# Second feed-forward: both transposes of a pair stand together on TensorE, the start of it is reordered on VectorE and ScalarE

## The chip, the cores and the metric

One core of one Trainium2 chip. The metric is device time in microseconds (us) of one execution, median of 3 runs. The profile is of one further execution, with its own time.

## The reference, cut to what matters

The output of a decayed linear attention (4 sequences, 768 positions, 8 heads of 64, so 3072 tokens of width 512) goes through two feed-forward stages. The second is the one that the change touches most:

```python
def _moe2_ref(x, w_in, w_out, g_ln):        # x 3072x512, w_in 512x1024, w_out 1024x512
    h = x @ w_in
    h_max = np.max(h, axis=-1, keepdims=True)
    e = np.exp(h - h_max)
    sm = e / (np.sum(e, axis=-1, keepdims=True) + 1e-09)
    solu = h * sm
    mu = np.mean(solu, axis=-1, keepdims=True)
    var = np.mean((solu - mu) ** 2, axis=-1, keepdims=True)
    ln = (solu - mu) / np.sqrt(var + 1e-06) * g_ln
    return (ln @ w_out).astype(np.float32)
```

The first one is `h = x @ w_in` (512 to 2048), ELU, `@ w_out`.

## The kernel before

Every engine has its program written out by hand; engines meet only at semaphores, and each engine works through its own list in order. So what stands ahead of an instruction in the list can hold it up even where its data are there. Matrix products are made in split precision: an operand is kept as a high half (ScalarE copies it) and a low half (GpSimd or VectorE subtracts), and each product is three matmuls. Up-projections use Winograd's form of Strassen's scheme: seven block products instead of eight, with sums before (GpSimd on the data, VectorE on the weights) and after.

The stages: attention in 12 steps; the first feed-forward in 3 blocks of 512 tokens by two, with 8 rounds `n` in each (`quadrants`, lines 882 and 1173; `up_pair` on TensorE); the second feed-forward in 12 pairs `u` of 128-token tiles `t` = 2u and 2u+1. Between the last two stages lies a passage, in which the last down-products of the first stage, the first pairs of the second and the writing back of results are woven by hand.

One pair `u` of the second feed-forward:

- TensorE makes seven block products of 6 matmuls each (128x512). In `opening_products` (L675): P1 (A11 B11) into PSUM bank X (4), P6 (S2 T2) into bank Y (5). In `middle_products` (L684): P2 (A12 B21) into X, P5 (S1 T1) into bank W (6), P7 (S3 T3) into Y. In `last_products` (L693): P4 (A22 T4) into Y, P3 (S4 B22) into W.
- ScalarE copies X after P1 (`copy_p1`, L1215) and after P2 (`copy_h2`, L1222). VectorE makes five sums out of SBUF and PSUM (`add`, L946): U2 from Y after P6, U3 from Y after P7, H22 = U3 + W after P5 (these three are `first_sums`, L948), H21 from Y after P4, H12 = U2 + W after P3 (`last_sums`, L958). P7 may not start before U2 has been read out of Y, P4 not before U3, P3 not before H22.
- For each tile: VectorE takes the row maximum (L978), ScalarE the exponential (L1235), VectorE the product (L985), statistics (L991 to L1005), GpSimd one power of -1/2 (`rstd`, L524), VectorE the normalisation (L1012 to L1016) into `e3`. TensorE transposes the tile in 8 transposes of 128x128 into banks 0 and 1 (`norm_transposes`, L743), ScalarE copies the high half out (`normalised_hi`, L1245), VectorE the low half (`normalised_lo`, L967), and TensorE multiplies with the second weight (`solu_down`, L757 to L759: two quarters `q` of 12 matmuls each for a tile).

TensorE's loop over p (L763) treats pair p+1's up-products together with pair p's tiles t = 2p, t+1. Its order before: opening and middle products of pair p+1; transposes of t; last products of p+1; transposes of t+1; four `solu_down` quarters. VectorE's order in the loop (L1041): `first_sums(p+1)`, low halves of t, `last_sums(p+1)`, maximum of t+2, low halves of t+1, maximum of t+3, then for t+2 and t+3 in turn product, statistics, normalisation. GpSimd (L536) splits the low halves of pair p+2 (L518, after ScalarE's copy L1228), sums those of p+3, and makes the two powers.

In round n = 0 of the first feed-forward, `keep_p1(1)` (ScalarE, L1171) and `keep_u2(1)` (VectorE) stand behind the high and low half of a quadrant (`split_g_hi`, `split_g_lo`); the second product of round 1 that adds to X waits for `keep_p1(1)`.

Of the kernel before, what the change touches and what calls it, by code (L numbers as in the profile page):

```python
# [6 lines left out]
B, H, S, D = 4, 8, 768, 64  # L7
# [43 lines left out]
def build(nc, units, w1, w_in2, w_out2, g_ln, tables, x_dram, x2_dram, out):  # L51
# [4 lines left out]
    with ctx:  # L56
# [31 lines left out]
        v_decay = place("v_decay", H, f32, CONST_AT + 32)  # L88
        state_decay = place("state_decay", H, f32, CONST_AT + 64)
# [50 lines left out]
        causal = place("causal", C, f32, E_AT + 2 * K2)  # L140
# [77 lines left out]
        v_decay_in = sem("v_decay_in")  # L218
        causal_in = sem("causal_in")
        state_decay_in = sem("state_decay_in")  # L220
# [61 lines left out]
        P1, P6, P2, P5, P7, P4, P3 = range(1, 8)  # L282
        M1, M6, M2, M7, M5, M4, M3 = range(1, 8)
        U2, U3, H22, H21, H12 = range(1, 6)
# [158 lines left out]
        def _(pool):  # L443
# [9 lines left out]
            def decay_state(s):  # L453
                pool.wait_ge(state_summed, kvs(s + 1))
                if s >= 1:

                    pool.wait_ge(att_done, s)
                nc.gpsimd.tensor_tensor(state[:, (s + 1) % 2].rearrange("p n h c -> p (n h) c"),
                                        state_sum[:, :].rearrange("p (h c) -> p h c", h=H),
                                        state_decay[:, :].unsqueeze(2).to_broadcast([P, H, D]), ALU.mult)\  # L460
                    .then_inc(state_done, 1)
# [20 lines left out]
            pool.wait_ge(state_decay_in, 16)  # L482
# [49 lines left out]
            sum_x2(2)  # L532
            split_x2_lo(2)
            rstd(0)
# [9 lines left out]
        def _(pe):  # L544
# [128 lines left out]
            X, Y, W = ps[:, 4, :], ps[:, 5, :], ps[:, 6, :]  # L673

            def opening_products(u):  # L675
                pe.wait_ge(x2l_done, 7 * (u + 1))
                if u > 0:
                    pe.wait_ge(h2_copied, u)
                up_product(u, X, A11, B11, True)
                if u > 0:  # L680
                    pe.wait_ge(h2_summed, sums(u - 1, H21))
                up_product(u, Y, S2, T2, True)

            def middle_products(u):  # L684
                pe.wait_ge(p1_copied, u + 1)
                up_product(u, X, A12, B21, False)
                if u > 0:
                    pe.wait_ge(h2_summed, sums(u - 1, H12))
                up_product(u, W, S1, T1, True)
                pe.wait_ge(h2_summed, sums(u, U2))  # L690
                up_product(u, Y, S3, T3, False)

            def last_products(u):  # L693
                pe.wait_ge(h2_summed, sums(u, U3))
                up_product(u, Y, A22, T4, False)
                pe.wait_ge(h2_summed, sums(u, H22))
                up_product(u, W, S4, B22, False)
# [39 lines left out]
            def norm_transposes(t):  # L737
                pe.wait_ge(soft[t % 2], SOFT * (t // 2 + 1))
                pe.wait_ge(nl_done, 2 * t)
                for q in range(2):  # L740
                    for f in range(NF2 // 2):
                        ff = q * (NF2 // 2) + f
                        last = nc.tensor.transpose(ps[:, q, f * P:(f + 1) * P], e3[:, t % 2, ff * P:(ff + 1) * P],  # L743
                                                   ident[:, :])
# [18 lines left out]
            for p in range(NPAIR - 1):  # L763
# [8 lines left out]
                norm_transposes(t)  # L772
                last_products(p + 1)
# [6 lines left out]
                else:  # L780
                    norm_transposes(t + 1)
# [14 lines left out]
        def _(dve):  # L796

            def apply_mask(s, one):
# [5 lines left out]
                table = causal[:, :].unsqueeze(1).to_broadcast([P, H, C])  # L804
# [40 lines left out]
            dve.wait_ge(causal_in, 16)  # L845
# [32 lines left out]
            def keep_u2(n):  # L878
                dve.wait_ge(p1_kept, n + 1)
                keep_sum(u2[:, :], n, U2, p1[:, n % 2, :], ps[:, up_bank(n // NFP) + 1, :], M6)  # L880

            def quadrants(n):
# [32 lines left out]
                split_g_lo(down_no(blk, 0, 2 * i + 1), e21)  # L915
                if n == 0:
                    keep_u2(1)
                activate(stash[:, 2 * i, :], n, G12, stash[:, 2 * i, :])
# [22 lines left out]
            X, Y, W = ps[:, 4, :], ps[:, 5, :], ps[:, 6, :]  # L941
# [6 lines left out]
            def first_sums(u):  # L948
# [3 lines left out]
                add(u3[:, :], u, U3, kept, Y, P7)  # L952
                dve.wait_ge(h2_summed, sums(u, U3))
                add(h2[:, 1, 512:1024], u, H22, u3[:, :], W, P5)
# [3 lines left out]
            def last_sums(u):  # L958

                add(h2[:, 1, 0:512], u, H21, kept, Y, P4)  # L960
                add(h2[:, 0, 512:1024], u, H12, u2[:, :], W, P3)

            def normalised_lo(t):
                for q in range(2):
                    dve.wait_ge(nh_done, 2 * t + q + 1)
                    part = slice(q * (NF2 // 2), (q + 1) * (NF2 // 2))
                    nc.vector.tensor_tensor(n_lo[:, t % 2, part, :], ps[:, q, :].rearrange("p (f t) -> p f t", t=P),  # L967
# [66 lines left out]
            add(h2[:, 1, 512:1024], 1, H22, u3[:, :], W, P5)  # L1034
            normalised_lo(0)
            solu_spread(1)
            solu_variance(1)
            add(h2[:, 1, 0:512], 1, H21, kept, Y, P4)
            solu_normalise(1)
            add(h2[:, 0, 512:1024], 1, H12, u2[:, :], W, P3)  # L1040
            for p in range(NPAIR - 1):  # L1041
                t, final = 2 * p, p == NPAIR - 2
                if p > 0:
                    if p > 1:
                        first_sums(p + 1)
                    normalised_lo(t)
                    last_sums(p + 1)
                if p > 0:
                    solu_max(t + 2)
                    normalised_lo(t + 1)  # L1050
                else:
                    normalised_lo(t + 1)
                    solu_max(t + 2)
# [8 lines left out]
                if p == 0:  # L1062

                    dve.wait_ge(p1_copied, 3)
                    add(u2[:, :], 2, U2, kept, Y, P6)
                solu_product(t + 3)
                solu_spread(t + 3)
                if p == 0:
                    add(u3[:, :], 2, U3, kept, Y, P7)
                solu_variance(t + 3)  # L1070
                if p == 0:
                    dve.wait_ge(h2_summed, sums(2, U3))
                    add(h2[:, 1, 512:1024], 2, H22, u3[:, :], W, P5)
# [6 lines left out]
        def _(act):  # L1080
            act.dma_start(v_decay[:, :], tables[:, T_VDEC:T_VDEC + H]).then_inc(v_decay_in, 16)
            act.dma_start(causal[:, :], tables[:, T_CAUSAL:T_CAUSAL + C]).then_inc(causal_in, 16)
            act.dma_start(state_decay[:, :], tables[:, T_SDEC:T_SDEC + H]).then_inc(state_decay_in, 16)
# [45 lines left out]
            act.wait_ge(v_decay_in, 16)  # L1129
# [43 lines left out]
            def quadrants(n):  # L1173
# [67 lines left out]
            def normalised_hi(t):  # L1241
                for q in range(2):
                    act.wait_ge(tr_done, 2 * t + q + 1)
                    part = slice(q * (NF2 // 2), (q + 1) * (NF2 // 2))
                    nc.scalar.activation(n_hi[:, t % 2, part, :], ps[:, q, :].rearrange("p (f t) -> p f t", t=P), ACT.Copy)\  # L1245
# [29 lines left out]
            split_x2_hi(2)  # L1275
            evacuate(NBLK - 1, 1)
            copy_p1(1)
            solu_exp(1)
            copy_h2(1)
            for p in range(NPAIR):  # L1280
# [7 lines left out]
                if p < NPAIR - 1:  # L1288
                    normalised_hi(t)
                normalised_hi(t + 1)  # L1290
                if p < NPAIR - 1:
                    solu_exp(t + 2)
                evacuate_y(t)
# [9 lines left out]
T_QDEC, T_CAUSAL, T_IDENT, T_VDEC, T_SDEC = 0, HH * C, HH * C + C, HH * C + C + P, HH * C + C + P + H  # L1303


def decay_tables():
# [8 lines left out]
    parts = [q_decay.reshape(P, HH * C), causal, np.eye(P), v_decay, state_decay]  # L1315
# [35 lines left out]
```

## Time and profile before

| | us |
|---|---|
| median of 3 runs | 846.46 (846.24 to 847.91) |
| the profiled execution | 846.25 |
| its span | 844.5 |
| TensorE busy in the span | 832.6 |
| VectorE busy | 551.6 |
| ScalarE busy | 418.6 |
| GpSimd busy | 391.9 |
| twelve pairs of the second feed-forward, from the first product to the end | 560.4 to 844.5 |
| the passage (first pairs, about) | 560 to 633 |

Busy shares are means over stages. A matmul's recorded duration overlaps the next one's, so the step from one start to the next is the better measure of it. A timeline gives the start, the duration, the engine, the line and, in brackets, how long the engine was idle before and what released it.

### The profile page before, as it was taken

Reading aid. Unit: us, or ns where it says so; the run is one execution under the profiler, and the core shown is the slowest. Engines: PE = TensorE matmul, PEld = TensorE weight load, DVE = VectorE, ACT = ScalarE, POOL = GpSimd, SP = SyncE. Lnnn points to the kernel's source line nnn. Section 1 sums busy time; section 2 is a strip of 40 time slices with the busy share of each in tenths; the row PEclk is TensorE's granted clock in tenths of the full one; section 3 lists DMA queues with packets and bytes.
Section 4 is the critical chain, followed back from the end, with each engine's and each line's share of the span. In section 5 each row is a group of like instructions: output and inputs, shape, how many; then the busy total and the mean of one; then the engine's idle time right before and its main releaser. Section 6 shows DMA issues by size and latency. Waiting matters only on the chain.

```text
span 844.5 us, 12593 instructions
## 1 busy us (share of the span) xinstructions
PE 832.6 (99%) x4853; PEld 690.6 (82%) x4853; DVE 551.6 (65%) x848; ACT 418.6 (50%) x678; POOL 391.9 (46%) x447
## 2 busy tenths in 40 slices
PE   8999999999999999999999999999999999999998
PEld 6898788888888888888888888887878888888886
DVE  3687767767634555575455555888877777777773
ACT  4685666565435555553455554653334433334422
POOL 3687766754025575710367570654353334344200
PEclk9999999999999999999999999999999999999999
DMA  9999400105012010140201003512011111111001
GB/s 352 403 398 339 174 26 27 48 26 178 1 33 67 26 50 26 57 142 1 75 26 51 25 26 99 158 59 85 25 50 50 50 50 49 40 51 50 25 14 50
DMA packets 49499, 73.57 MB, mean 87 GB/s; under 512 B 3232, under 2 KB 23968, under 8 KB 49184
## 3 DMA queue, kind: packets, MB, share of 16 engines
q1 hardware_dynamic: 49008, 72.69, 25.1%
q8 instruction: 39, 0.64, 0.3%
q14 instruction: 20, 0.16, 0.1%
q10 hardware_dynamic: 432, 0.07, 0.1%
HBM read 55.98 MB, written 16.78 MB: 86 GB/s over the span
## 4 chain that ended last, share of the span: by engine, by line
PE 91%; DVE 5%; DMA 1%; ACT 1%; SPq 1%; issue 0%; POOL 0%; DVEq 0%; ACTq 0%
PE ps L656 10%; PE ps L657 10%; PE ps L660 10%; PE ps L609 9%; PE ps L611 9%; PE ps L610 9%; PE ps L757 5%; PE ps L758 5%; PE ps L759 5%; PE ps L668 4%; PE ps L670 4%; PE ps L669 4%; PE ps L586 2%; PE ps L743 2%; PE ps L561 2%; DMA k<-units_dram 1%
## 5 line engine op out<-in xcount | busy, mean ns | idle before, releaser
L479 POOL TENSOR_TENSOR u_lo<-u_raw,u_hi 128x256 fp32r<-128x256 f32 x168 | 141.9, 878 | 192.9 <-ACT u_hi L1113 192.9
L657 PE MATMUL ps<-g_hi,wd_lo 128*128 128x512 f32 x384 | 149.4, 389 | 0.0
L656 PE MATMUL ps<-g_hi,wd_hi 128*128 128x512 f32 x384 | 149.4, 389 | 0.0
L660 PE MATMUL ps<-g_lo,wd_hi 128*128 128x512 f32 x384 | 149.4, 389 | 0.0
L609 PE MATMUL ps<-x_hi,u_hi 128*128 128x512 f32 x336 | 131.3, 391 | 0.8 <-ACT p L1171 0.8
L610 PE MATMUL ps<-x_hi,u_lo 128*128 128x512 f32 x336 | 130.8, 389 | 0.0
L611 PE MATMUL ps<-x_lo,u_hi 128*128 128x512 f32 x336 | 130.7, 389 | 0.0
L474 POOL TENSOR_TENSOR u_raw<-u_raw 128x256 f32<-128x256 f32 x96 | 88.6, 923 | 16.7 <-DMA u_raw<-w_dram 10.8
L660 PEld LDWEIGHTS ps<-g_lo,wd_hi 128*128 128x128 f32 x384 | 72.1, 188 | 15.0
L656 PEld LDWEIGHTS ps<-g_hi,wd_hi 128*128 128x128 f32 x384 | 72.1, 188 | 15.0
L657 PEld LDWEIGHTS ps<-g_hi,wd_lo 128*128 128x128 f32 x384 | 72.1, 188 | 14.9
L518 POOL TENSOR_TENSOR u_lo<-x_raw,u_hi 128x256 fp32r<-128x256 f32 x84 | 66.2, 821 | 22.6 <-ACT u_hi L1228 22.6
L757 PE MATMUL ps<-wd_hi,n_hi 128*128 128x512 f32 x192 | 75.8, 395 | 0.2 <-DVE n_lo L967 0.2
L609 PEld LDWEIGHTS ps<-x_hi,u_hi 128*128 128x128 f32 x336 | 63.1, 188 | 15.3 <-ACT p L1171 1.9
L759 PE MATMUL ps<-wd_hi,n_lo 128*128 128x512 f32 x192 | 74.8, 390 | 0.0
L758 PE MATMUL ps<-wd_lo,n_hi 128*128 128x512 f32 x192 | 74.8, 389 | 0.0
L611 PEld LDWEIGHTS ps<-x_lo,u_hi 128*128 128x128 f32 x336 | 63.1, 188 | 13.1
L610 PEld LDWEIGHTS ps<-x_hi,u_lo 128*128 128x128 f32 x336 | 63.1, 188 | 12.9
L668 PE MATMUL ps<-x_hi,u_hi 128*128 128x512 f32 x168 | 66.9, 398 | 0.0
L524 POOL TENSOR_TENSOR stats<-stats,minus_half 128x1 f32<-128x1 f32 x24 | 13.2, 551 | 115.5 <-DVE stats L1005 115.5
L670 PE MATMUL ps<-x_hi,u_lo 128*128 128x512 f32 x168 | 65.6, 391 | 0.0
L669 PE MATMUL ps<-x_lo,u_hi 128*128 128x512 f32 x168 | 65.4, 389 | 0.0
(87 smaller groups left out, 1486.2 us busy)
## 6 DMA issues: line engine op xcount, KB each, us to landing
u_raw<-w_dram SPq DMA_DIRECT2D x24, 512.0 KB, 3.5
q<-units_dram SPq DMA_DIRECT2D x12, 512.0 KB, 6.5
v<-units_dram SPq DMA_DIRECT2D x12, 512.0 KB, 7.5
k<-units_dram SPq DMA_DIRECT2D x12, 512.0 KB, 8.2
x_between<-x SPq DMA_DIRECT2D x24, 256.0 KB, 2.7
x_raw<-x_between SPq DMA_DIRECT2D x12, 512.0 KB, 3.5
out_dram<-y_sb SPq DMA_DIRECT2D x24, 256.0 KB, 2.0
kn<-units_dram SPq DMA_DIRECT2D x10, 512.0 KB, 8.9
```

Source lines behind the costliest of these rows:

```text
L479: nc.gpsimd.tensor_tensor(u_lo[n % 2][:, o, :], u_raw[n % 2][:, o, :], u_hi[n % 2][:, o, :].bitcast(f32), ALU.subtract).then_inc(ul_done, 1)
L609: nc.tensor.matmul(bank, hi, x_hi[:, b, k, :], start=(first and k == 0), stop=False, skip_group_check=True)
L610: nc.tensor.matmul(bank, lo, x_hi[:, b, k, :], start=False, stop=False, skip_group_check=True)
L611: done = nc.tensor.matmul(bank, hi, x_lo[:, b, k, :], start=False, stop=(k == 1), skip_group_check=True)
L656: nc.tensor.matmul(ps[:, bank + m, :], hi, g_hi[:, no % 3, :], start=(f == 0), stop=False)
L657: nc.tensor.matmul(ps[:, bank + m, :], lo, g_hi[:, no % 3, :], start=False, stop=False)
L660: last = nc.tensor.matmul(ps[:, bank + m, :], hi, g_lo[:, no % 3, :], start=False, stop=(f == NF1 - 1))
L668: nc.tensor.matmul(bank, x_h, hi, start=(first and k == 0), stop=False, skip_group_check=True)
L670: done = nc.tensor.matmul(bank, x_l, hi, start=False, stop=(k == 1), skip_group_check=True)
L757: nc.tensor.matmul(bank, n_hi[:, par, f, :], hi, start=(f == 0), stop=False)
L758: nc.tensor.matmul(bank, n_hi[:, par, f, :], lo, start=False, stop=False)
L759: last = nc.tensor.matmul(bank, n_lo[:, par, f, :], hi, start=False, stop=(f == NF2 - 1))
```

## The change

Three things are done. First, three small tables (a causal mask and two decay tables) are loaded by one DMA and awaited by one semaphore. Second, in round 0 of the first feed-forward `keep_p1(1)` moves ahead of the wait for `g_done` on ScalarE, and `keep_u2(1)` ahead of `split_g_lo` on VectorE. Third, in the second feed-forward:

- For pairs u = 3 and on the seven products run in the order P1, P6, P2, P7, P5, P4, P3; P5 and P3 use bank 4 (X) instead of 6, so P5 waits for `copy_h2(u)` and P1 of the next pair for H12.
- For p = 3 and on both transposes stand ahead of the last products; odd tiles from t = 5 on are transposed into banks 6 and 7 and wait for older low halves.
- VectorE's order in the loop for p of 2 and more is as it was. What lies ahead of it, and p = 0, is written out anew: product and statistics of tile 0 ahead of the evacuation, low halves of tile 1 behind the maxima of 2 and 3 and the product and statistics of tile 2, U3 and H22 of pair 2 behind the normalisation of tile 3.
- ScalarE takes the exponential of tile 1 ahead of the evacuation, the high halves of pair 2 (`split_x2_hi(2)`) behind `copy_p1(1)`, and in p = 0 the exponential of tile 2 and `evacuate_y(0)` ahead of the high halves of tile 1. GpSimd makes `rstd(0)` ahead of `split_x2_lo(2)`.

```diff
+        P1, P6, P2, _, _, P4, P3 = range(1, 8)
+        def separate(u):
+            return u < 3
+        def P5(u):
+            return 4 if separate(u) else 5
+        def P7(u):
+            return 5 if separate(u) else 4
+        def w_bank(u):
+            return 6 if separate(u) else 4
+        def normed_bank(t):
+            return 0 if t < 4 else 6 * (t % 2)
@@ GpSimd
+            rstd(0)
             split_x2_lo(2)
-            rstd(0)
@@ opening_products
+                if u > 0 and not separate(u - 1):
+                    pe.wait_ge(h2_summed, sums(u - 1, H12))
@@ middle_products
-                if u > 0:
-                    pe.wait_ge(h2_summed, sums(u - 1, H12))
-                up_product(u, W, S1, T1, True)
+                if separate(u):
+                    if u > 0:
+                        pe.wait_ge(h2_summed, sums(u - 1, H12))
+                    up_product(u, ps[:, w_bank(u), :], S1, T1, True)
                 pe.wait_ge(h2_summed, sums(u, U2))
                 up_product(u, Y, S3, T3, False)
+                if not separate(u):
+                    pe.wait_ge(h2_copied, u + 1)
+                    up_product(u, ps[:, w_bank(u), :], S1, T1, True)
@@ norm_transposes
-                pe.wait_ge(nl_done, 2 * t)
+                if t == 5:
+                    pe.wait_ge(h2_summed, sums(2, H12))
+                else:
+                    pe.wait_ge(nl_done, 2 * t if t <= 4 else 2 * (t - 1))
@@ TensorE's loop over p
                 norm_transposes(t)
+                if not separate(p):
+                    norm_transposes(t + 1)
                 last_products(p + 1)
...
-                    norm_transposes(t + 1)
+                    if separate(p):
+                        norm_transposes(t + 1)
                     solu_down(t, 0)
@@ VectorE, ahead of its loop
+            solu_product(0)
+            solu_spread(0)
+            solu_variance(0)
             evacuate(NBLK - 1, 1)
-            solu_product(0)
+            solu_normalise(0)
             dve.wait_ge(p1_copied, 2)
             add(u2[:, :], 1, U2, kept, Y, P6)
-            solu_spread(0)
-            solu_variance(0)
-            solu_normalise(0)
-            add(u3[:, :], 1, U3, kept, Y, P7)
             solu_product(1)
+            add(u3[:, :], 1, U3, kept, Y, P7(1))
...
+            solu_max(2)
+            solu_max(3)
+            solu_product(2)
+            solu_spread(2)
+            normalised_lo(1)
+            solu_variance(2)
+            solu_normalise(2)
+            dve.wait_ge(p1_copied, 3)
+            add(u2[:, :], 2, U2, kept, Y, P6)
+            solu_product(3)
+            solu_spread(3)
+            solu_variance(3)
+            solu_normalise(3)
+            add(u3[:, :], 2, U3, kept, Y, P7(2))
@@ ScalarE, round 0 of the first feed-forward
+                if n == 0:
+                    keep_p1(1)
                 act.wait_ge(g_done, quads(n, G21))
                 split_g_hi(down_no(blk, 0, 2 * i + 1), e21)
-                if n == 0:
-                    keep_p1(1)
@@ tables
+            act.dma_start(decays[:, :], tables[:, T_DECAYS:T_DECAYS + C + 2 * H]).then_inc(decays_in, 16)
-            act.dma_start(v_decay[:, :], tables[:, T_VDEC:T_VDEC + H]).then_inc(v_decay_in, 16)
-            act.dma_start(causal[:, :], tables[:, T_CAUSAL:T_CAUSAL + C]).then_inc(causal_in, 16)
-            act.dma_start(state_decay[:, :], tables[:, T_SDEC:T_SDEC + H]).then_inc(state_decay_in, 16)
```

## Rows read from the trace of the kernel before

**Rows 1.** The page, part 1 (busy time) and the granted clock of part 2.

```profile
PE 832.6 (99%) x4853; PEld 690.6 (82%) x4853; DVE 551.6 (65%) x848; ACT 418.6 (50%) x678; POOL 391.9 (46%) x447
...
PEclk9999999999999999999999999999999999999999
```

**Rows 2.** Busy time of each engine in one steady pair, then granted clock, DMA.

```profile
744.67:767.07 22.40, 22.40 (x107) 18.58 (x106) 16.75 (x35) 8.53 (x13) 8.95 (x14) 1.00 0.13 48
```

**Rows 3.** TensorE's timeline around both transposes of p = 7 (start, duration).

```profile
744.67 1.04 PE L743 MATMUL ps<-ident,e 128*128 128x128 f32 x8
745.62 0.50 PE L668 MATMUL ps<-x_hi,u_hi 128*128 128x512 f32 x1
745.95 0.40 PE L669 MATMUL ps<-x_lo,u_hi 128*128 128x512 f32 x1
...
748.50 1.03 PE L743 MATMUL ps<-ident,e 128*128 128x128 f32 x8
749.29 0.48 PE L757 MATMUL ps<-wd_hi,n_hi 128*128 128x512 f32 x1
749.60 0.40 PE L758 MATMUL ps<-wd_lo,n_hi 128*128 128x512 f32 x1
```

**Rows 4.** VectorE's timeline, same pair: U3, H12, normalisation, U2 of the next.

```profile
744.87 0.69 DVE L946 TENSOR_TENSOR u<-p,ps 128x512 f32<-128x512 f32 x1 [3.15 <-PE ps L670]
...
748.70 0.69 DVE L946 TENSOR_TENSOR h<-u,ps 128x512 f32<-128x512 f32 x1 [0.62 <-PE ps L670]
...
757.21 0.16 DVE L1012 TENSOR_TENSOR stats<-stats 128x1 f32<-128x1 f32 x1 [0.66 <-POOL stats L524]
...
762.72 0.81 DVE L1016 TENSOR_SCALAR e<-e,stats 128x1024 f32<-128x1024 f32 x1
763.45 0.68 DVE L946 TENSOR_TENSOR u<-p,ps 128x512 f32<-128x512 f32 x1
```

**Rows 5.** ScalarE's and GpSimd's timelines of a steady pair: copies of X, low halves.

```profile
739.42 0.60 ACT L1215 ACTIVATE p<-ps 128x512 f32<-128x512 f32 x1 [0.70 <-PE ps L670]
...
742.14 0.60 ACT L1222 ACTIVATE h<-ps 128x512 f32<-128x512 f32 x1 [0.53 <-PE ps L670]
...
741.69 4.89 POOL L518 TENSOR_TENSOR u_lo<-x_raw,u_hi 128x256 fp32r<-128x256 f32 x7 [1.85 <-ACT u_hi L1228]
```

**Rows 6.** TensorE's timeline at the points of the passage and the first steady pairs.

```profile
584.63 0.39 PE L670 MATMUL ps<-x_hi,u_lo 128*128 128x512 f32 x1
586.43 1.06 PE L743 MATMUL ps<-ident,e 128*128 128x128 f32 x8 [1.42 <-DVE e L1016]
...
599.21 0.39 PE L757 MATMUL ps<-wd_hi,n_hi 128*128 128x512 f32 x1
...
614.06 1.06 PE L743 MATMUL ps<-ident,e 128*128 128x128 f32 x8 [1.30 <-DVE n_lo L967]
...
648.27 0.39 PE L668 MATMUL ps<-x_hi,u_hi 128*128 128x512 f32 x1
...
658.90 1.03 PE L743 MATMUL ps<-ident,e 128*128 128x128 f32 x8
```

**Rows 7.** VectorE's timeline in the passage, two instructions beside busy GpSimd.

```profile
579.46 1.71 DVE L985 TENSOR_TENSOR e<-e,h 128x1024 f32<-128x1024 f32 x1
...
592.50 0.69 DVE L1012 TENSOR_TENSOR stats<-stats 128x1 f32<-128x1 f32 x1
```

**Rows 8.** Round 1 of the first feed-forward: TensorE's and ScalarE's timelines.

```profile
93.35 0.50 PE L609 MATMUL ps<-x_hi,u_hi 128*128 128x512 f32 x1 [0.83 <-ACT p L1171]
...
92.18 0.63 ACT L1160 ACTIVATE g_hi<-e 128x512 fp32r<-128x512 f32 x1 [1.35 <-DVE e L865]
```

**Rows 9.** The page, part 3: the queue of the small tables.

```profile
q10 hardware_dynamic: 432, 0.07, 0.1%
```

**Rows 10.** TensorE's timeline near the end: transposes of tiles 21 and 22.

```profile
815.70 1.03 PE L743 MATMUL ps<-ident,e 128*128 128x128 f32 x8
...
825.17 1.09 PE L743 MATMUL ps<-ident,e 128*128 128x128 f32 x8 [0.27 <-DVE e L1016]
```

More of the change, by code:

```diff
@@ L878, in keep_u2 @@
             def keep_u2(n):
+                if n > 0:
+                    dve.wait_ge(h_summed, sums(n - 1, H12))
                 dve.wait_ge(p1_kept, n + 1)
@@ L914, in quadrants @@
                 activate(e21, n, G21, h21)
-                split_g_lo(down_no(blk, 0, 2 * i + 1), e21)
                 if n == 0:
                     keep_u2(1)
+                split_g_lo(down_no(blk, 0, 2 * i + 1), e21)
                 activate(stash[:, 2 * i, :], n, G12, stash[:, 2 * i, :])
@@ L951, in first_sums @@
                 add(u2[:, :], u, U2, kept, Y, P6)
-                add(u3[:, :], u, U3, kept, Y, P7)
+                add(u3[:, :], u, U3, kept, Y, P7(u))
                 dve.wait_ge(h2_summed, sums(u, U3))
-                add(h2[:, 1, 512:1024], u, H22, u3[:, :], W, P5)
+                add(h2[:, 1, 512:1024], u, H22, u3[:, :], ps[:, w_bank(u), :], P5(u))
             first_sums(0)
@@ L960, in last_sums @@
                 add(h2[:, 1, 0:512], u, H21, kept, Y, P4)
-                add(h2[:, 0, 512:1024], u, H12, u2[:, :], W, P3)
+                add(h2[:, 0, 512:1024], u, H12, u2[:, :], ps[:, w_bank(u), :], P3)
             def normalised_lo(t):
@@ L1033, in _ @@
             dve.wait_ge(soft[1], 3)
-            add(h2[:, 1, 512:1024], 1, H22, u3[:, :], W, P5)
+            dve.wait_ge(h2_summed, sums(1, U3))
+            add(h2[:, 1, 512:1024], 1, H22, u3[:, :], ps[:, w_bank(1), :], P5(1))
             normalised_lo(0)
             solu_spread(1)
+            add(h2[:, 1, 0:512], 1, H21, kept, Y, P4)
             solu_variance(1)
-            add(h2[:, 1, 0:512], 1, H21, kept, Y, P4)
+            add(h2[:, 0, 512:1024], 1, H12, u2[:, :], ps[:, w_bank(1), :], P3)
@@ L1039, in _ @@
             solu_normalise(1)
-            add(h2[:, 0, 512:1024], 1, H12, u2[:, :], W, P3)
-            for p in range(NPAIR - 1):
-                t, final = 2 * p, p == NPAIR - 2
[L1043 to L1053, printed above, removed]
+            solu_max(2)
@@ new lines, in _ @@
+            solu_max(3)
[11 more added lines that the diff above has]
+            add(u3[:, :], 2, U3, kept, Y, P7(2))
+            dve.wait_ge(h2_summed, sums(2, U3))
+            add(h2[:, 1, 512:1024], 2, H22, u3[:, :], ps[:, w_bank(2), :], P5(2))
@@ L1054, in _ @@
+            for p in range(1, NPAIR - 1):
+                t, final = 2 * p, p == NPAIR - 2
+                if p > 1:
+                    first_sums(p + 1)
+                normalised_lo(t)
+                last_sums(p + 1)
+                solu_max(t + 2)
+                normalised_lo(t + 1)
                 if not final:
@@ L1289, in _ @@
                     normalised_hi(t)
+                if p == 0:
+                    solu_exp(t + 2)
+                    evacuate_y(t)
                 normalised_hi(t + 1)
-                if p < NPAIR - 1:
+                if 0 < p < NPAIR - 1:
                     solu_exp(t + 2)
-                evacuate_y(t)
+                if p > 0:
+                    evacuate_y(t)
                 if p < NPAIR - 1:
```

48 lines of the change are left out of this document (18 added, 30 removed).

## The prediction, written before the changed kernel ran

> **What bounds the kernel now.** I read the page's busy shares first, then TensorE's waits, then busy time pair by pair, then the timelines. TensorE is busy 99% of the span at full granted clock [rows 1], so only two things can pay: its gaps, or its own work. Its waits are few; those of the second feed-forward stand at the transposes, behind VectorE's normalisation or low halves [rows 6]. In the seven pairs from 655 on, each 22.40 us long to 0.01, TensorE has no gap and VectorE is busy 16.75 us [rows 2]. That says TensorE is the bound there. It does not say how far VectorE is from being it: VectorE works in one long chain in order, and the edges by which TensorE and VectorE wait for each other decide. So the round through both engines has to be added up.
>
> **Units.** A 128x512 matmul costs 0.2267 us from start to start (a block product 1.36, a quarter of solu_down 2.72). Eight transposes cost 0.88: from 748.50 to the second matmul behind them at 749.60 are 1.10, less one matmul; nothing is lost on leaving them [rows 3]. The first group of a pair costs 0.18 more (744.67 to 745.95 less 1.10): P4 waits for U3, which starts 0.20 after P7's end and takes 0.69; it ends at 745.56, and P4's second matmul at 745.95 puts P4's nominal start at 745.72, so 0.16 from VectorE's end to TensorE [rows 3, 4].
>
> **Steady pairs, what goes.** With P7 ahead of P5, U3 is long there when P4 comes: 0.18 a pair goes. Standing together saves nothing else, as leaving costs nothing. P5 must now wait for X's copy: it takes 0.60 from P2's end [rows 5], under P7's 1.36, so nothing. The first of the two new waits on H12 has four quarters of cover (10.9 us).
>
> **Steady pairs, what comes.** P7 waits for U2. Before, P2 and P5 (2.72 us) stood between P6 and P7; now only P2. And from P3, which releases H12, to P7 the path on TensorE loses P5 (1.36) and one group of transposes (0.88). VectorE's chain from H12 to U2 keeps its order: it starts 0.20 after P3's end (748.50 to 748.70), U2 starts at 763.45, 14.75 later, and takes 0.68 [rows 3, 4]. I take this round for all seven. The only idle in it are two waits of 0.66 for GpSimd's power, which stay. From P3's end to P7's possible start: 0.20 + 14.75 + 0.68 + 0.16 = 15.79. TensorE's work between: four quarters 10.88, P1, P6, P2 4.08, together 14.96 (before: 0.88 + 14.96 + 1.36 = 17.20, so 1.4 to spare). So TensorE will stand 0.83 in front of P7. The round is then 15.79 + P7 and P5 2.72 + sixteen transposes 1.76 + P4 and P3 2.72 + 0.04 for a few matmuls recorded at 0.24 = 23.03, against 22.40: +0.63. It applies to pairs 5 to 11, seven rounds: +4.4. Bounds: 0.1 a round either way, 3.7 to 5.1; that margin is mine.
>
> **First steady pairs and passage.** All positions on the clock of before. The transposes of tile 0 stood at 586.43 where 584.86 was due (584.63 + 0.23), so 1.57 late, of which the row calls 1.42 idle [rows 6]. After: the product of tile 0 starts at about 576.4, when its exponential is done, not at 579.46 behind the evacuation, and escapes the 1.71 that it took there [rows 7], since GpSimd's low halves of pair 2 come later; statistics, evacuation (1.3), normalisation end near 582, 3 us early. Transposes at 584.86, then P4 waits for U3 (585.05 + 0.69 + 0.16 = 585.90). P4, P3, two quarters (8.2) lead to transposes of tile 1 at 594.06, P1 and P6 of pair 2 to 597.66. There solu_down of tile 1 wants low halves that now stand behind two maxima, a product and statistics (5.4 together): normalisation of tile 1 ends near 592.4, so they come at 597.85 and 598.45: wait 0.9, start 598.6 against 599.21 [rows 6]. Gain so far 0.6. Two quarters and P2, P5, P7 put the transposes of tile 2 at 608.1, P4 at 609.2, P3's end at 611.95. Low halves of tile 2 are done at 610.9, as nothing but H22 is ahead of them, so transposes of tile 3 start at 611.95 where they stood at 614.06: gain 2.1. In p = 2 the wait on U3 goes: P1 of pair 4 starts at 645.96 against 648.27, gain 2.3. Its U2 (H12 at 634.4 + 14.75 + 0.68 + 0.16 = 650.0, 0.2 more if GpSimd is in the way) and P7 (645.96 + 4.08 = 650.04) are level; I take 0.1 lost. The end of P3 of pair 4 then is 650.1 + 2.72 + 1.76 + 2.76 = 657.34 against 658.90: 1.56 gained (a group of transposes now lies ahead of it). Bounds 0.5 to 2.3, since each VectorE step here may run beside GpSimd.
>
> **The end.** Transposes of tile 22 follow the last P3's end (815.70) by 9.47, set by VectorE's chain (0.27 of it idle), not by TensorE's own 9.04 (0.88 + three quarters) [rows 10]. That chain stays, so they follow by 9.47 again: nothing given back; the group of transposes moved ahead of P3 is paid for there.
>
> **First feed-forward.** TensorE waits in round 1 for keep_p1(1): P2 starts at 93.35 after 0.83 idle, by the 0.15 of the same kind as at 584.63 some 1.0 late (due 92.36), and 0.1 is lost behind it. ScalarE stood idle from 90.83 to 92.18 [rows 8]. P1 of this round ended one product (P6) ahead of 92.36, at 91.0, and its copy of 0.6 can end at 91.8. U2 of round 1 then is done at 93.2 for its product at 93.7. Gain 1.1 (0.9 to 1.1); no wait of TensorE follows for 160 us that could eat it. The added wait in keep_u2 is for a sum that VectorE made itself, earlier: nothing. It delays split_g_lo by 0.4, with 2.5 to its use.
>
> **Tables.** Three DMAs become one: 256 packets fewer of 432 on that queue (128 rows each). Its share, 0.05 to 0.15% of 16 engines' 844.5 us, is 16 to 47 ns a packet [rows 9]; 256 of them over 16 engines are 0.25 to 0.75 us of the loads at the start, of which TensorE need not see all. I take 0.2 (0 to 0.6). The merged table, about 5 us to land by its issues at the start, comes ahead of the first value load that ScalarE waits for anyway.
>
> **Sum.** +4.4 - 1.56 - 1.1 - 0.2 = +1.54. On the profiled execution: 846.25 + 1.54 = 847.8; on the median, 0.21 above it: 848.0.
>
> **A rule weighed.** A small instruction of VectorE with two SBUF inputs took 0.69 instead of 0.16, beside GpSimd's work [rows 4, 7]. The Trainium skill, SBUF — State Buffer, section "Who interferes with whom", says that VectorE and GpSimd share one port pair as a lock, and that the one who issues first holds it while the other blocks. By it, what counts is who starts first.
>
> **Rivals.** *The forecast* (VectorE's chain sets the round): 0.62, its own range 846.4 to 849.6.
>
> *TensorE stays the bound* (faster). For it: VectorE is busy only 16.75 of 22.40 [rows 2]; against it: 15.79 is longer than 14.96. It needs the chain to be 0.8 shorter, which nothing in its order gives. Then the 2.3 gained by pair 4 stand, eight pairs gain 0.18 each (1.4), the end takes back the 0.88 of the transposes moved ahead of P3, and 1.3 come from the first feed-forward and the tables: 2.3 + 1.4 - 0.9 + 1.3 = 4.1 off, so 842.3. 0.10. Half a stall (chain shorter by 0.4, a price of 0.3 less in seven rounds) gives 845.9: 0.12.
>
> *GpSimd's low halves enter VectorE's chain* (clearly slower). In a round they start 2.3 after ScalarE's copy of X (739.42 to 741.69) [rows 5]; with P1 now ending earlier against the chain, that is 14.53 after H12, while L1012 of the second tile stands at 13.57 and L1016 from 14.02 to 14.83. If they come 1 us earlier, L1012 costs 0.53 more (0.69 for 0.16 [rows 4, 7]): 3.7 in seven rounds, so 851.7. It decides from a start ahead of 13.57; the sum leaves 0.96. 0.06. By the lock of the Trainium skill, L1016 begins first at 14.02 and keeps its 0.81, and GpSimd waits. A milder form counts here too: the passage gives nothing because low halves of tile 1 come over 2 us late: 849.6 or more. 0.10.
>
> **How the numbers follow.** What a measurement of this kernel can tell from no change is about 0.2%, 1.7 us: 844.8 to 848.2. The forecast lies just inside; with the bounds of its terms (3.7 to 5.1, 0.5 to 2.3, 0 to 0.6) its 0.62 splits into about 0.32 within and 0.30 above. Half a stall adds 0.10 within and 0.02 below, the faster rival 0.10 below, the slower ones 0.16 above. Faster 0.12, same 0.42, slower 0.46. The range leaves out the faster rival and the worst of the slower one: 844.6 to 850.2.
>
> **What would show it.** Steady pairs of 23.0 with a TensorE gap of about 0.6 to 0.8 ahead of P7 (S3 T3), released by VectorE's L946 sum u, seven times; VectorE's H12 to U2 still 14.75; no gap ahead of P4. Tile 0's transposes without gap; tile 1's solu_down with about 0.7 behind low halves; tile 3's without gap. Round 1 without gap. The prediction is wrong if pairs are 22.2 (no gap: the chain was shorter) or above 23.3 (L1012 or L1016 slow).

## The result and the profile after

The changed kernel takes 850.56 us (median of 6 runs, 850.43 to 852.41), against 847.12 us for the kernel before on the same chip (6 runs, 846.24 to 849.88): a ratio of 1.0041, with a 95% interval of 1.0025 to 1.0056, so 3.4 us slower (2.1 to 4.7). The forecast was 848.0 with a range up to 850.2. Slower by over 0.2% was the case with the largest chance, but the forecast time itself was 2.6 too low.

The profiled execution of after took 851.77 us, with a span of 850.0; the profiled one of before took 846.25, with 844.5 [rows 1]. Their difference of 5.5 is more than the 3.4 of the medians: this execution of after lies 1.2 above its median, the one of before 0.9 below its own. How far the start can scatter between executions is shown below.

The page of after, part 1 and the granted clock of part 2 (against rows 1), and its queue of small tables (against rows 9: now 144 packets for 432):

```profile
PE 834.7 (98%) x4853; PEld 692.7 (81%) x4853; DVE 553.8 (65%) x848; ACT 418.4 (49%) x678; POOL 393.6 (46%) x447
...
PEclk8999999999999999999999999999999999999999
...
q10 hardware_dynamic: 144, 0.07, 0.0%
```

TensorE's waits in after (line, releaser: us in total, times, longest):

```profile
PE ps L683 <- DVE u L976: 4.0, 7, 0.6
PE ps L576 <- DMA k<-units_dram: 3.1, 1, 3.1
...
PE ps L767 <- DVE e L1046: 1.2, 1, 1.2
...
PE ps L781 <- DVE n_lo L997: 0.7, 2, 0.5
PE ps L624 <- ACT p L1204: 0.6, 1, 0.6
```

Four readings follow, in the order of their size. The first row is new and is the forecast's stall: seven waits in front of P7, released by the sum u (U2). The second is TensorE's wait for the first keys, longer by 1.6 than in before, where one such wait was 1.5. The waits in front of the transposes of tiles 0 and 3 [rows 6] are gone; what is left under L767 is the one at the end. And a wait for ScalarE's p in the first feed-forward is still there, but in another round.

**A steady pair.** TensorE's timeline of after at the end of pair 5 (start, duration, idle before and its releaser), against rows 3:

```profile
674.61 0.39 PE L685 MATMUL ps<-x_hi,u_lo 128*128 128x512 f32 x1
675.57 0.50 PE L683 MATMUL ps<-x_hi,u_hi 128*128 128x512 f32 x1 [0.57 <-DVE u L976]
...
678.42 1.91 PE L767 MATMUL ps<-ident,e 128*128 128x128 f32 x16
680.09 0.48 PE L683 MATMUL ps<-x_hi,u_hi 128*128 128x512 f32 x1
...
821.21 0.39 PE L781 MATMUL ps<-wd_hi,n_hi 128*128 128x512 f32 x1
...
830.68 1.09 PE L767 MATMUL ps<-ident,e 128*128 128x128 f32 x8 [1.16 <-DVE e L1046]
```

P7 starts 0.96 behind the last matmul of P2 where 0.23 would be due: 0.73 lost, and about 0.1 more in the matmuls behind it. The row itself calls only 0.57 idle, since the modelled end of a matmul lies 0.39 after its start. The sixteen transposes stand together and no gap is left in front of P4. Busy time of the next pair (stretch, length, then busy time of PE, PEld, DVE, ACT, POOL, granted clock, DMA share, GB/s), against rows 2:

```profile
678.42:701.46 23.04, 22.47 (x107) 18.51 (x106) 16.95 (x35) 8.43 (x13) 9.17 (x14) 1.00 0.13 46
```

A pair takes 23.04 (23.03 to 23.07 in all seven) for 22.40, though VectorE is busy only 16.95 of it. VectorE's timeline of the same pair shows what set it (against rows 4): H12, the first step of the chain, and U2, its last.

```profile
683.11 0.69 DVE L976 TENSOR_TENSOR h<-u,ps 128x512 f32<-128x512 f32 x1 [0.67 <-PE ps L685]
...
691.62 0.16 DVE L1042 TENSOR_TENSOR stats<-stats 128x1 f32<-128x1 f32 x1 [0.66 <-POOL stats L539]
...
697.14 0.81 DVE L1046 TENSOR_SCALAR e<-e,stats 128x1024 f32<-128x1024 f32 x1
697.87 0.68 DVE L976 TENSOR_TENSOR u<-p,ps 128x512 f32<-128x512 f32 x1
```

From 683.11 to 697.87 are 14.76, with no wait for TensorE in between. TensorE follows VectorE in one place of the round and VectorE follows TensorE in one, and the sum of the two sets its length.

**The span in five stretches**, each from the same event in both profiled executions. "Due" is the start that the first transposes would have had without a wait.

| Stretch | before | after | difference | predicted |
|---|---|---|---|---|
| start to the first product of the first feed-forward | 77.07 | 79.93 | +2.86 | -0.2 |
| from there to the due start of the transposes of tile 0 | 507.79 | 507.60 | -0.19 | -1.1 |
| from there to the end of P3 of pair 4 | 74.04 | 72.35 | -1.69 | -1.56 |
| seven steady rounds | 156.80 | 161.33 | +4.53 | +4.4 |
| P3's last end to the end of the span | 28.8 | 28.8 | 0 | 0 |

So the three terms of the second feed-forward were right to 0.15 us each, and the two terms ahead of them were wrong.

**The start.** TensorE's timeline of before and of after, first 13 us:

```profile
1.31 5.43 PE L701 MATMUL ps<-warm 128*128 128x512 bf16 x13 [1.31 <-POOL warm L444]
8.24 2.06 PE L561 MATMUL ps<-q,k 64*128 64x128 f32 x32 [1.50 <-DMA k<-units_dram]
```

```profile
1.31 4.53 PE L722 MATMUL ps<-warm 128*128 128x512 bf16 x13 [1.31 <-POOL warm L459]
8.98 3.78 PE L576 MATMUL ps<-q,k 64*128 64x128 f32 x32 [3.13 <-DMA k<-units_dram]
12.69 1.97 PE L589 MATMUL ps<-v,kn 128*64 128x64 f32 x32
```

The same 32 score matmuls take 2.06 in before and 3.78 in after. The windows of 5 to 10 and 10 to 15 us say why (columns as above), before first:

```profile
5.00:10.00 5.00, 3.50 (x35) 2.21 (x35) 1.77 (x3) 2.45 (x8) 0.00 (x0) 1.00 1.05 393
10.00:15.00 5.00, 4.68 (x97) 4.35 (x95) 2.83 (x4) 2.92 (x10) 3.37 (x2) 1.00 1.06 409
```

```profile
5.00:10.00 5.00, 1.87 (x13) 1.22 (x13) 1.29 (x2) 2.44 (x8) 0.00 (x0) 0.79 1.00 336
10.00:15.00 5.00, 5.00 (x66) 4.78 (x66) 2.73 (x3) 2.18 (x9) 2.36 (x1) 0.53 1.05 409
```

In before the keys land at 8.2, 1.5 after the last warm-up matmul, and the granted clock stays at full speed, the level of 2.4 GHz. In after they land at 9.0, 3.1 after it, and the clock is at half speed, the level of 1.2 GHz, for the first 5.7 us of real work: read in narrower windows, it is at 0.50 from 8.0 to 14.7 and at 1.00 from 14.8. Two things differ ahead of that: the keys land 0.7 later, and the warm-up ends 0.9 earlier. The second has to do with no DMA that the change touches, as far as these runs tell. The 13 warm-up matmuls start 0.427 apart at first and 0.216 apart once the clock has risen. In after that comes behind the eighth of them, in before only with the last. In the other executions it came between 4.0 and 6.7 us, with one table DMA and with three alike.

**The first feed-forward.** The wait of round 1 [rows 8] is gone: P2 follows P6 at once, at 95.19. But one round later TensorE waits where it did not before:

```profile
109.92 0.39 PE L626 MATMUL ps<-x_lo,u_hi 128*128 128x512 f32 x1
110.90 0.50 PE L624 MATMUL ps<-x_hi,u_hi 128*128 128x512 f32 x1 [0.59 <-ACT p L1204]
```

GpSimd's and ScalarE's timelines of after lead back from there:

```profile
97.14 3.04 POOL L489 TENSOR_TENSOR u_raw<-u_raw 128x256 f32<-128x256 f32 x3 [1.51 <-DMA u_raw<-w_dram]
```

```profile
101.03 1.71 ACT L1146 ACTIVATE u_hi<-u_raw 128x1792 fp32r<-128x1792 f32 x1 [1.60 <-POOL u_raw L489]
```

GpSimd's sums of the weights of round 2 wait 1.51 for their DMA, ScalarE's split of them waits 1.60 for GpSimd, and the copy that releases P2 is queued behind that split. The load is queued on SyncE behind fourteen loads of the down weights.

### The profile page after: what moved, and what is told of

Read it like the earlier page. It is cut to its first block, busy times and chain, and to the rows that moved or that the text cites. A ratio compares the mean times of both kernels' runs of the same rounds, so it can differ in the third digit from the quotient of the medians.

```text
span 850.0 us, 12591 instructions
## 1 busy us (share of the span) xinstructions
PE 834.7 (98%) x4853; PEld 692.7 (81%) x4853; DVE 553.8 (65%) x848; ACT 418.4 (49%) x678; POOL 393.6 (46%) x447
## 4 chain that ended last, share of the span: by engine, by line
PE 80%; DVE 14%; issue 2%; DMA 2%; POOL 1%; ACT 1%; SPq 0%; DVEq 0%; ACTq 0%; POOLq 0%
PE ps L671 10%; PE ps L672 10%; PE ps L675 10%; PE ps L624 9%; PE ps L625 8%; PE ps L626 8%; PE ps L683 3%; PE ps L685 3%; PE ps L684 3%; PE ps L576 3%; PE ps L601 3%; DVE bn L1025 3%; DVE stats L1008 3%; DVE e L1015 2%; PE ps L767 2%
```

## The experiments

Two theories of the steady rounds: A, VectorE's chain from H12 to U2 sets the round, as forecast; B, standing together or the new banks cost TensorE something by themselves. Two of the start: C, the merged table DMA has to do with the late keys and the lowered clock; D, it varies from execution to execution and the profile of after was bad luck. All ratios are to the kernel before, run beside the kernel on the same chip. All of these kernels compute the whole result.

### Transposes apart again, new order of products kept

```diff
                 norm_transposes(t)
-                if not separate(p):
-                    norm_transposes(t + 1)
                 last_products(p + 1)
...
-                    if separate(p):
-                        norm_transposes(t + 1)
+                    norm_transposes(t + 1)
                     solu_down(t, 0)
```

> The changed kernel, but the two groups of transposes stand apart again for p of 3 and more (before and behind the last products); P7 stays ahead of P5. Theory (VectorE's chain of 15.8 from P3's end to P7 sets the round, and standing together took 0.88 of cover out of it): TensorE then has 0.88 + 14.96 = 15.84 in that stretch, level with the chain, P4 no longer waits for U3: steady pairs of 22.2 to 22.35, the gap ahead of P7 gone or under 0.1, time about 844.0. Rival (the swap of P5 and P7 alone costs it, since U2 has only one product of cover): pairs stay at 22.9 to 23.1 with the gap of 0.6, time about 850.

Measured: 844.89 us (843.33 to 846.70, 11 runs), ratio 0.9971 (0.9959 to 0.9983). The list of TensorE's waits has none ahead of P7, and one of the steady pairs is

```profile
700.77:722.99 22.22, 22.22 (x108) 18.54 (x106) 16.84 (x35) 8.53 (x13) 8.74 (x14) 1.00 0.14 48
```

The seven take 22.22 to 22.45, 22.32 in the mean. Eight transposes (0.88) put back between P3 and P7 give TensorE enough to do while the chain runs, or nearly: the expectation had 15.84 of work level with a chain of 15.8, and in the longest pairs some 0.2 is still lost at P7 (its first matmuls at 697.91 and 787.15). So the pairs are 0.08 shorter than before's 22.40 in the mean, and 0.18, what the forecast gave to P7 ahead of P5, only in the shortest. The first transposes to those of tile 22 take 237.20, against 243.15 in after. Standing together is what costs, but this run can't tell whether by the chain or by itself.

### Transposes together, U2 ahead of the last normalisation

```diff
                 if final:
                     normalised_lo(NT - 2)
+                else:
+                    dve.wait_ge(p1_copied, p + 3)
+                    add(u2[:, :], p + 2, U2, kept, Y, P6)
                 solu_normalise(t + 3)
...
-                dve.wait_ge(p1_copied, u + 1)
-                add(u2[:, :], u, U2, kept, Y, P6)
+                if u == 0:
+                    dve.wait_ge(p1_copied, u + 1)
+                    add(u2[:, :], u, U2, kept, Y, P6)
                 add(u3[:, :], u, U3, kept, Y, P7(u))
```

> The changed kernel, but VectorE makes U2 of the next pair ahead of the normalisation of tile t+3 instead of behind it (p of 1 to 9), in the time in which it waits for GpSimd's power. Transposes still together. Theory (the chain up to U2 is the bound): U2 then ends at 14.3 instead of 15.4 after H12, before P7 wants to start, the gap ahead of P7 goes and pairs fall from 23.06 to about 22.2, time about 844.6. Rival (transposes together cost by themselves, on TensorE): pairs stay above 22.8.

Measured: 844.15 us (842.06 to 846.57, 6 runs), ratio 0.9964 (0.9951 to 0.9978). This is the test that separates A from B, for here the transposes stand together in the new banks. A pair, and U2 in VectorE's timeline:

```profile
678.40:700.57 22.17, 22.17 (x108) 18.59 (x107) 17.25 (x35) 8.43 (x13) 9.40 (x14) 1.00 0.13 48
```

```profile
696.75 0.69 DVE L976 TENSOR_TENSOR u<-p,ps 128x512 f32<-128x512 f32 x1 [0.71 <-PE ps L685]
697.35 0.15 DVE L1043 TENSOR_TENSOR stats<-stats 128x1 f32<-128x1 f32 x1
...
697.79 1.08 DVE L1047 TENSOR_SCALAR e<-e,stats 128x1024 f32<-128x1024 f32 x1
```

The releaser has changed sides: U2 now waits for TensorE, and no longer TensorE for U2. It starts 13.67 after H12 (683.08), where it started 14.76 after it, and the 22.17 are TensorE's own work. B falls: together costs nothing by itself. On the way, L1047 takes 1.08 where the same step took 0.81 in after; VectorE has room for that here.

### Passage of after, steady pairs of before

```diff
         def separate(u):
-            return u < 3
+            return True
...
-            return 0 if t < 4 else 6 * (t % 2)
+            return 0
...
-                if t == 5:
-                    pe.wait_ge(h2_summed, sums(2, H12))
-                else:
-                    pe.wait_ge(nl_done, 2 * t if t <= 4 else 2 * (t - 1))
+                pe.wait_ge(nl_done, 2 * t)
```

> The changed kernel with the steady pairs as before: P5 ahead of P7 in bank 6, transposes apart, all in banks 0 and 1; the passage, the first feed-forward and the tables as changed. Theory: pairs of 22.40 with no gap ahead of P7, passage as in the changed kernel, so 7 x 0.66 + 0.88 - 2 x 0.18 = 5.1 us below it, about 845.4, and 1.8 to 2.3 us below the kernel before at equal starts. Rival (the passage gains nothing once the start is taken out): about 847.5.

Measured: 844.78 us (843.01 to 846.11, 6 runs), ratio 0.9964 (0.9951 to 0.9977). Pairs take 22.38 to 22.42, and the first transposes to those of tile 22 take 238.03, against 240.31 of before (from 584.86, where they were due, to 825.17 [rows 10]): the passage gives 2.3, as the forecast's sum had it up to pair 4. The steady pairs of after take back 5.1 (243.15 less 238.03), as expected.

### The three table DMAs put back, and the single one in the kernel before

```diff
-            act.dma_start(decays[:, :], tables[:, T_DECAYS:T_DECAYS + C + 2 * H]).then_inc(decays_in, 16)
+            act.dma_start(v_decay[:, :], tables[:, T_VDEC:T_VDEC + H]).then_inc(v_decay_in, 16)
+            act.dma_start(causal[:, :], tables[:, T_CAUSAL:T_CAUSAL + C]).then_inc(causal_in, 16)
+            act.dma_start(state_decay[:, :], tables[:, T_SDEC:T_SDEC + H]).then_inc(state_decay_in, 16)
```

> The changed kernel with the three small tables loaded by three DMAs again, all else as changed. Theory A (the single table DMA is what made the start worse: the first keys land later against the end of the warm-up matmuls, TensorE idles 3.1 us instead of 1.5 and the granted clock falls to 0.5 to 0.8 until 15 us): the start goes back to the old one, granted clock of the run 1.00 instead of 0.996 to 0.998, time 1.5 to 2.9 us below the changed kernel, about 848.3. Theory B (the start varies by itself, or by the code's other changes): time and clock as in the changed kernel, 850.5 within 0.5.

> The kernel before with nothing changed but the single table DMA. Theory A (the table DMA costs the start): 1.5 to 2.9 us slower than the kernel before, granted clock 0.996 to 0.998. Theory B (it does not): within 0.5 us of the kernel before, clock as there; by the prediction's own term it would even gain 0.2.

Measured: after with three DMAs 849.67 us (848.63 to 850.71, 6 runs), ratio 1.0031 (1.0020 to 1.0042); before with one DMA 848.84 us (846.72 to 850.50, 11 runs), ratio 1.0017 (1.0007 to 1.0026). The second interval excludes zero: the single DMA costs 1.4 us here (0.6 to 2.2), where I had forecast a gain of 0.2. The first run settles nothing: its clock is 1.00 in two of six runs and 0.998 in four, its time lies between both theories (848.3 and 850.5), and its interval overlaps that of after (1.0025 to 1.0056). The profiled execution of before with one DMA has nearly the same start as that of after:

```profile
8.85 3.79 PE L558 MATMUL ps<-q,k 64*128 64x128 f32 x32 [3.03 <-DMA k<-units_dram]
```

```profile
10.00:15.00 5.00, 5.00 (x68) 4.78 (x66) 2.87 (x3) 2.38 (x9) 2.36 (x1) 0.53 1.06 408
```

But C alone doesn't hold. The mean granted clock of an execution tells how much of the start ran at the lower level. It was 0.996 to 0.997 in 6 of 11 runs of this kernel and in 5 of 24 of before. So D is true of both, and the single DMA may make it more frequent, on few runs. The 24 runs of before have a median of 847.38 and reach from 846.12 to 850.05, the ten at 1.00 or 0.999 from 846.12 to 847.87. By what path one DMA fewer would make the start slower no run shows.

### First feed-forward as before

```diff
                 exponent(n, G21, p1[:, n % 2, :])
-                if n == 0:
-                    keep_p1(1)
                 act.wait_ge(g_done, quads(n, G21))
                 split_g_hi(down_no(blk, 0, 2 * i + 1), e21)
+                if n == 0:
+                    keep_p1(1)
...
-                if n == 0:
-                    keep_u2(1)
                 split_g_lo(down_no(blk, 0, 2 * i + 1), e21)
+                if n == 0:
+                    keep_u2(1)
```

> The changed kernel with keep_p1(1) and keep_u2(1) of the first feed-forward put back behind the halves of the quadrant. Theory (the wait of round 1 was traded for one of round 2, on data whose load lands late): the gap of 0.8 at P2 of round 1 returns, the gap of 0.6 at P2 of round 2 goes, and the time from the first product of the first feed-forward to the first transposes grows by 0.3 only, the whole time by 0 to 0.5. Rival (the prediction: the 1.1 us of round 1 are gained whole, and the new wait comes from something else): that stretch grows by 1.1.

Measured: 852.26 us (851.06 to 853.25, 4 runs), ratio 1.0052 (1.0035 to 1.0069). The whole time says little, since in its profiled execution the keys came at 9.90, after 3.78 idle, and the scores ran slow; the stretch counts. It has the gap of round 1 again and none at round 2:

```profile
97.44 0.50 PE L624 MATMUL ps<-x_hi,u_hi 128*128 128x512 f32 x1 [0.86 <-ACT p L1204]
```

From the first product to the due start of the first transposes it takes 507.85, the length that it has in before (507.79), against 507.60 in after. So this part of the change gives 0.25 between these two executions, where 1.1 was forecast: in after the wait wasn't removed, it moved one round on. This run alone doesn't prove it. GpSimd had its weights of round 2 here at 16.19 us behind the first product, against 17.21 in after, so they were early for any order. The traces with the old order and late weights close that hole: in before with one table DMA (17.07) and in before with 22 warm-up matmuls (16.98) TensorE has no wait at round 2, and both stretches are 507.87. With the new order the wait follows the landing. P2 of round 2 starts 0.2 late at 16.36 and 16.67, 0.5 at 16.83 and 16.86, 0.7 at 17.10 and 17.21, and 1.1 at 17.89 (after with 22 warm-up matmuls).

### A longer warm-up

```diff
-WARM = 13
+WARM = 22
```

> The changed kernel with 22 warm-up matmuls instead of 13, so that TensorE is busy until 7.8 to 8.7 us instead of 5.8 to 6.8. Theory A (the start costs more when TensorE idles 2 to 4 us for the first keys and the granted clock then falls to 0.5 for the first attention step): the run's granted clock is 1.00 in most runs, no run at 0.996, the times bunch near the changed kernel's good start, 848.3 to 849.0. Theory B (late keys alone cost it, not the clock): the keys land as late as before, times stay near 850.5.

> U2 made early on VectorE and 22 warm-up matmuls, the rest as changed. Theory: both gains add: pairs of 22.18, granted clock 1.00, about 842.3, 4.5 to 5 us below the kernel before. Rival (longer warm-up only delays the first scores): 844 or more.

> The kernel before with 22 warm-up matmuls instead of 13 and nothing else. Theory (the spread of the kernel before, 846.1 to 850.4, comes from its start, where TensorE's clock falls in some runs while it waits for the first keys): no run below a granted clock of 0.999, the median 0.5 to 1.0 below that of the kernel before, and the slow runs from 848.5 on gone. Rival (the warm-up was long enough, the spread is the loads' alone): same median and spread.

| Kernel | us, median (range, runs) | ratio (95%) |
|---|---|---|
| after, 22 warm-up matmuls | 849.39 (848.40 to 851.61, 12) | 1.0022 (1.0011 to 1.0033) |
| U2 early, 22 | 843.01 (842.40 to 844.10, 5) | 0.9949 (0.9937 to 0.9962) |
| before, 22 | 846.92 (846.26 to 847.57, 10) | 0.9978 (0.9969 to 0.9987) |

With it the granted clock is 1.00 or 0.999 in all runs but one. The kernel before loses its longer times: against its own 14 runs on that chip its spread falls from 3.4 us to 1.3, its median from 848.47 to 846.92, and the ratio makes it 1.9 faster (interval 1.1 to 2.6). The direction was as expected, the size was expected at 0.5 to 1.0. U2 early with 22 came out 0.7 above its forecast of 842.3. TensorE is idle for 0.97 between the warm-up and the scores, and those take 2.06:

```profile
1.31 6.25 PE L701 MATMUL ps<-warm 128*128 128x512 bf16 x22 [1.31 <-POOL warm L444]
8.54 2.06 PE L561 MATMUL ps<-q,k 64*128 64x128 f32 x32 [0.97 <-DMA k<-units_dram]
```

The clock is not all of the start. After with 22 was expected at 848.3 to 849.0 and still had runs up to 851.4 at a clock of 1.00, and in its profiled execution (849.6 span) the keys landed at 10.37, after 1.71 idle, with the clock at 1.00. Why keys land anywhere between 8.2 and 10.6 with the same loads issued was not found.

### Both, with three tables; and the load of round 2 moved forward

```diff
             for f in range(2, NF1):
                 load_wd(f)
+                if f == 7:
+                    load_u(2)
...
-                    if NFP * blk + i + 2 < NU:
+                    if 2 < NFP * blk + i + 2 < NU:
```

> U2 early, 22 warm-up matmuls, and three DMAs for the small tables again. Theory A (the single table costs the start through the clock only, by shifting when keys land against the warm-up): with the clock held it makes no difference, 843.0 within 0.4. Theory B (the single table also delays the keys by themselves): 0.5 to 1.0 faster than with the single table, about 842.3.

> U2 early, 22 warm-up matmuls, and the weights of round 2 of the first feed-forward (512 KB) are asked for after six of the fourteen weight loads that stood ahead of them on SyncE's queue, not after all. Theory (the wait of 0.4 to 0.9 at P2 of round 2 is there because these weights land late): the gap at P2 of round 2 is gone, and the time from the first product of the first feed-forward to the first transposes is 507.0 to 507.1 as in the runs that had no such gap, time about 842.6. Rival (the gap comes from ScalarE's own order): it stays.

Measured, both on top of U2 early and 22 warm-up matmuls: with three table DMAs 842.88 us (842.77 to 844.73, 5 runs), ratio 0.9937 (0.9923 to 0.9951); with the load moved (one table) 842.68 us (842.41 to 843.80, 5 runs), ratio 0.9933 (0.9920 to 0.9945). With the clock held, the number of table DMAs makes no difference that these runs can tell. The moved load does what it should: GpSimd's sums of round 2 no longer wait,

```profile
93.61 4.36 POOL L491 TENSOR_TENSOR u_raw<-u_raw 128x256 f32<-128x256 f32 x4
```

TensorE waits in neither round, and the stretch to the first transposes is 506.65 (from 77.96 to 584.61), against 507.32 in the version with three tables and in U2 early with 22: 0.67 less. It is 1.14 less than before's 507.79, which is the whole of the 1.1 forecast for this part. The whole time shows only 0.2 of the 0.67, within what the start scatters. This last kernel is 0.67% faster than the one before.

## Why the prediction was wrong

**The steady pairs: right.** Forecast 23.03 a round, a stall of 0.83, H12 to U2 14.75; measured 23.03 to 23.07, 0.73 and 0.1 behind it, 14.76. Seven rounds, +4.5 for +4.4. The chain as the cause is shown, not only read: putting 0.88 of TensorE's work back under it leaves at most 0.2 of the stall, and taking one normalisation out of it, with the transposes left together, removes the stall whole.

**The passage: right in sum, right in most of its steps.** Transposes of tiles 0 and 3 without gap. solu_down of tile 1 at 601.01 waited 0.46 (0.6 lost) where 0.9 was forecast. -1.69 for -1.56.

**The end: right.** From P3's last end (821.21) to the transposes of tile 22 (830.68) are 9.47, as before.

**The first feed-forward: wrong, 0.9 us.** The first failed step is the sentence "no wait of TensorE follows for 160 us that could eat it". That was true of before, where round 2 started late enough for its weights. With TensorE and ScalarE a microsecond earlier, the weights of round 2 were late: GpSimd's row in before shows that it already waited for them there, for 0.64, and the prediction had not looked at it:

```profile
93.38 3.53 POOL L474 TENSOR_TENSOR u_raw<-u_raw 128x256 f32<-128x256 f32 x4 [0.64 <-DMA u_raw<-w_dram]
```

Where they happened to land earlier two thirds of the gain came: 507.08 with three tables and 507.03 with the passage only, against 507.79 in before. With the load moved forward all of it came: 506.65. So the 1.1 of round 1 was sized rightly; what the sum lacked is the next wait behind it, for the weights of round 2.

**The tables: wrong sign, about 1.0 us at the median.** The second failed step is this term. It was costed as packets saved at the start, by the time a packet takes (288 went, not the 256 of the sum; that changes little). What the start goes by is when the first keys land and how long TensorE has been idle by then. The trace of before showed 1.50 of idle time ahead of the first scores, and the bounds (0 to 0.6 gained) left out a loss. Taking the stretches of the profiled pair off the difference of the medians leaves 3.44 + 1.69 + 0.19 - 4.53 = +0.8 for the start. The runs with one table in the kernel before show +1.4 (0.6 to 2.2), which agrees. How the single DMA does it stays open: with 22 warm-up matmuls one table and three gave 843.01 and 842.88. The Trainium skill, TensorE: Matmul & The Clock Gate, section "What's actually happening", says that an idle TensorE falls back to the lower clock. The traces agree: with 1.50 idle the clock stayed at 1.00, with 3.13 idle it had fallen before the scores began, and was at 0.53 in the window of 10 to 15 us. The prediction had no rival for it.

**The base: 0.66 us.** The median of before was 846.46 from three runs and is 847.12 from six, those three among them. Three runs of a kernel that scatters over 4 us were taken as exact.

The whole miss at the median is 850.56 - 848.0 = 2.56 = 0.66 (base) + 0.9 (first feed-forward) + 1.0 (start). The last term is what is left over at the median, so it also holds whatever else the start did there. The rivals played no part: GpSimd didn't enter VectorE's chain in after (its low halves start 14.50 after H12, forecast 14.53, and L1046 kept its 0.81), and TensorE wasn't the bound.

## What to carry to other kernels

Before work is moved out of a place, add up the round through both engines from each release to the next: an engine that is busy 75% of a round can set it when its chain runs in order. Here 1.4 us were to spare; moving one product (1.36) used them up, and the 0.88 of "free" work moved with it became the stall. A removed wait is a gain only as far as the next step in order that waits for a DMA; follow it there, also on the engines that feed it. Where a kernel's time scatters, look at the granted clock at the start first, and keep TensorE busy until the first data land.

## What the runs showed of the hardware

- After a warm-up of 4.5 to 7.3 us, TensorE's granted clock was 1.00 in the window of 10 to 15 us with 0.8 to 1.7 us idle behind the warm-up (five executions with a wait, idle times 0.79, 0.97, 1.05, 1.50, 1.71). With 2.00 idle (two executions) it was 0.66 in that window, with 3.03 and 3.13 it was 0.53, with 3.46 to 4.40 it was 0.50. The length of the warm-up and the moment at which the clock rose differ between them too, so the idle time isn't varied alone. Gaps of 0.57 once every 23 us later on left it at 1.00.
- 13 warm-up matmuls took 4.50 to 5.59 us in different executions, by where in it the step fell from 0.427 to 0.216: behind the eighth of them at the earliest, not at all at the latest. The clock column reads 1.00 there from the start, also where the matmuls are 0.427 apart: ahead of the first change on record it tells nothing, and the steps have to be read. The first keys landed between 8.2 and 10.6. The runs of after with 22 warm-up matmuls scatter over 3 us at a clock of 1.00.
- VectorE's last normalisation L1046 of after starts at 697.14 and keeps its 0.81, though GpSimd's low halves start at 697.61, before its end. With U2 moved, the same step starts at 697.79, behind GpSimd's start at 697.59, and takes 1.08. GpSimd pays too: its first low half takes 0.93 in after, and with U2 moved the one that starts during L1047 takes 1.18, where others take 0.73. The rule of the Trainium skill that the prediction weighed (SBUF — State Buffer, "Who interferes with whom": the one who issues first holds the port) would have it so. Two pairs of rows agree with it, and no run varied this by itself.
